# Gate logits on VectorE instead of TensorE, the second square on ScalarE, and two buffers instead of three in a fused attention and mixture-of-experts kernel

## The chip, the cores and the metric

The kernel runs on one core of a Trainium2 chip. The metric is the device time of one execution in microseconds (us). TensorE is called PE in the profile, VectorE DVE, ScalarE ACT, GpSimd POOL, and SyncE, which issues most of the DMAs, SP.

## The reference

Three stages follow one another, all in float32:

```python
kv  = einsum('bhsd,bhse->bhde', k, v)            # 8 batches, 8 heads, 576 positions, 64 wide
out = einsum('bhsd,bhde->bhse', q, kv)
x   = out / sqrt(mean(out*out, -1) + 1e-6) * g_norm    # -> [4608, 512]
y   = (maximum(x @ w_in, 0) ** 2) @ w_out              # 512 -> 2048 -> 512
logits = y @ w_gate + modality_bias[modality_id]       # [4608, 8], 8 experts
e, gate = argmax(logits), softmax(logits)[argmax]
out[token] = gate * (maximum(y @ w1[e], 0) @ w2[e])    # 512 -> 1024 -> 512
```

## The kernel before

The 4608 tokens are cut into twelve groups of 384 (three tiles of 128). During group m, TensorE computes y for group m. Woven into it are the attention of group m+1 ("attend", tasks of `ATTEND`) and the gate routing of group m-1 ("route", tasks of `ROUTE`). After the groups, token rows are fetched by expert in tiles of 128 and multiplied by w1 and w2 (`tile`, L832). That second part takes about 510 us and is not touched by the change, except that its first tile also routes group 11.

A group has sixteen chunks c of 128 hidden columns. TensorE's order is fixed: F(c) (`first_product`, L636: twelve matmuls of 384 columns into one of two PSUM banks `ps_h`), then the tasks at place 2c, then S(c-2) (`second_product`, L649: nine matmuls of 512 columns into `ps_y`), then the tasks at place 2c+1; S(14) and S(15) close the group. Each product is split in a high and a low part, so both operands exist twice. Between F(c) and S(c) the hidden values pass through ScalarE and VectorE: relu (L979), high part of the square (`g_hi`, L981), both on ScalarE; the exact square (`g_sb`, L1203) and the low part (`g_lo`, L1208) on VectorE. `g_hi` and `g_lo` have three buffers each.

ScalarE and VectorE take the other tasks of places 2c-1 and 2c within chunk c, on ScalarE after `g_hi(c)`, on VectorE between the exact square and `g_lo(c)`. The tasks of one attention tile t are qT (four transposes of q, copied by ScalarE), heads (products with kv, then a square on ScalarE L934, then on VectorE a sum L1082, twelve small steps of an inverse root, and a scaling L1065 into `xn`), and xT (four transposes of `xn`, a ScalarE copy L937, a VectorE subtraction L1088). Places: heads 16, 21, 26; xT 20, 25, 30. The kv products are made for the attention of group m+1 by four tasks (L668) at places 5, 7, 9 and 11; groups 1, 4, 7 and 10 have none, since their next group uses those already made, and are shorter.

The routing of a group: yT at places 2, 5, 8 (four transposes of y, copied by ScalarE, L943), logits at 4, 7, 10 (four products with `w_gate`, L717), then argmax, gate and prefix as small VectorE steps with one pair of products (L724, L726). From the prefix come list entries that GpSimd scatters to DRAM (L550).

Beside this the expert weights are split into high and low parts, twelve pieces of 128x512 in a group (eight in the last): SP loads a piece, ScalarE rounds it (L922, last work of its chunk), GpSimd subtracts (L543), SP stores both parts. There are two stage buffers, so a load waits for a store of two pieces before. In group 0, w_in and w_out go the same way.

ScalarE and VectorE are in order: a task that waits holds all behind it.

Of the kernel before, what the change touches and what calls it, by code (L numbers as in the profile page):

```python
# [30 lines left out]
P = 128  # L31
# [32 lines left out]
def routed_mlp_program(nc, q, k, v, g_norm, w_in, w_out, modality, w_gate, bias, w1, w2, out):  # L64
# [22 lines left out]
    ROUTE = [(2, "yT", 0), (3, "bias", 0), (4, "logits", 0), (5, "yT", 1), (7, "logits", 1), (8, "yT", 2),  # L87
             (10, "logits", 2), (12, "argmax", 0), (13, "gate", 0), (14, "prefix", 0)]
# [4 lines left out]
    PREPARE = [(24, "early", 0), (27, "rows", 0)]  # L93
# [5 lines left out]
    rows_dram = nc.dram_tensor("rows", [N + 1, ROW], F32, kind="Internal").ap()  # L99
    lists_dram = nc.dram_tensor("lists", [EARLY * P + E * LIST, 1], F32, kind="Internal").ap()  # L100

    with ExitStack() as ctx:
# [13 lines left out]
        with nc.sbuf_tensor("first_loads", [P, 4, KC * GROUP], F32) as first_loads:  # L116
            pass
        xT = {n: [sb(f"xT{n}_{part}", [P, KC, GROUP], F32R) for part in ("hi", "lo")] for n in (1, 2, 0)}
# [7 lines left out]
        g_sb = sb("g_sb", [P, GROUP])  # L126
        g_hi = [sb(f"g_hi{n}", [P, GROUP], F32R) for n in range(3)]
        g_lo = [sb(f"g_lo{n}", [P, GROUP], F32R) for n in range(3)]
# [35 lines left out]
        k_first = k_sb + [first_loads[0:SP, 2 + n, 0:K_V].rearrange("p (j h d) -> p j h d", j=SJ, h=PAIR) for n in range(2)]  # L164
        v_first = v_sb + [first_loads[0:SP, 2 + n, K_V:2 * K_V].rearrange("p (h j d) -> p h j d", h=PAIR, j=SJ)
                          for n in range(2)]
        q_first = [q_sb[:, :]] + [first_loads[:, n, 0:D] for n in range(2)]
        qT_first = [tile_T[:, :, :]] + [stage_hi[n][:, :].bitcast(F32).rearrange("p (k t) -> p k t", t=P) for n in range(2)]
        norm_first = g_sb[:, 0:6 * TILES * H].rearrange("p (n h) -> p n h", n=6)
# [28 lines left out]

        def chunks(ap):
            return ap.rearrange("p (k t) -> p k t", t=P)  # L200
# [9 lines left out]
        stage_out = [sem(f"stage_out{n}") for n in range(2)]  # L210
        lists_set, rows_out, lists_in, row_in, scattered = (
# [1113 lines left out]
```

## Time and profile before

| | us |
|---|---|
| three executions | 1524.31, 1529.36, 1524.43 (median 1524.43) |
| span of the profiled execution | 1524.2 |
| PE busy | 1478.5 (97%) |
| DVE busy | 619.1 (41%) |
| ACT busy | 498.7 (33%) |
| POOL busy | 365.0 (24%) |
| mean granted TensorE clock | 0.990 |

The span is the time from the first to the last instruction of the one profiled execution; it is 0.2 us below the median. The end of group m is seen where y is copied out of PSUM (L1215): at 123.0, 200.7, 283.3, 366.9, 444.2, 526.9, 610.3, 687.9, 770.6, 854.1, 930.9 and 1011.9 us for groups 0 to 11. In timelines the first number is the start and the second the duration, both in us; a release in brackets is the idle time ahead and what ended it.

### The profile page before, as it was taken

The page shows a single profiled execution, that of the slowest core. Times are in us where ns is not written, and L with a number is a line of the kernel's source. Part 1 is how long each engine was busy: PE and PEld are TensorE (multiplying, and loading weights), DVE is VectorE, ACT ScalarE, POOL GpSimd, SP SyncE. Part 2 cuts the span into 40 slices and gives each one's busy share as a digit, 9 for nine tenths or more (in the row PEclk, how much of TensorE's full clock was granted, in tenths as well). Part 3 has the DMA queues.
Part 4 walks back from the last instruction along what each step waited for, and adds up shares of the span by engine and source line. Part 5 has one row for each costly group of instructions (what it writes and reads, how often), then busy time and mean ns, then how long its engine had stood idle before and what let it go on. Part 6 is the DMA issues. An engine that isn't in the chain of part 4 may idle for free.

```text
span 1524.2 us, 24645 instructions
## 1 busy us (share of the span) xinstructions
PE 1478.5 (97%) x7915; PEld 1301.5 (85%) x7916; DVE 619.1 (41%) x1538; ACT 498.7 (33%) x927; POOL 365.0 (24%) x377
## 2 busy tenths in 40 slices
PE   6899999999999999999999999988999999999998
PEld 5788998988999998999898999876888888888886
DVE  3363635445554535453636464422222222222222
ACT  2343433433433333433333433321222222222222
POOL 2452312121312122222222131202222222222221
PEclk8999999999999999999999999999999999999999
DMA  6633655563656463464655354754875112751170
GB/s 155 162 101 118 171 173 162 154 183 92 201 123 209 106 194 123 153 170 156 162 171 160 111 180 151 217 199 156 319 284 182 41 41 78 268 213 41 47 255 21
DMA packets 192772, 236.42 MB, mean 155 GB/s; under 512 B 92287, under 2 KB 107039, under 8 KB 192674
## 3 DMA queue, kind: packets, MB, share of 16 engines
q1 hardware_dynamic: 185122, 215.18, 46.1%
q0 software_dynamic: 7552, 20.03, 3.9%
q8 instruction: 50, 0.82, 0.3%
q14 instruction: 48, 0.39, 0.1%
HBM read 148.14 MB, written 88.07 MB: 155 GB/s over the span
## 4 chain that ended last, share of the span: by engine, by line
PE 85%; DMA 6%; DVE 3%; issue 3%; POOL 2%; ACT 1%; SPq 1%; DVEq 0%; POOLq 0%; ACTq 0%
PE ps_y L810 15%; PE ps_h L810 14%; PE ps_h L632 7%; PE ps_y L632 7%; PE ps_h L634 7%; PE ps_h L633 7%; PE ps_y L634 7%; PE ps_y L633 7%; PE ps_a L668 2%; PE ps_b L695 2%; PE ps_b L717 2%; DMA stage<-in_moe_w_in 2%; DMA w_lo<-stage 1%; PE ps_c L755 1%; PE ps_y L823 1%
## 5 line engine op out<-in xcount | busy, mean ns | idle before, releaser
L543 POOL TENSOR_TENSOR stage<-stage,stage_hi 128x512 f32<-128x512 f32 x128 | 167.6, 1309 | 652.9 <-ACT stage_hi L922 575.0
L1203 DVE TENSOR_TENSOR g_sb<-relu_sb 128x384 f32<-128x384 f32 x192 | 131.5, 685 | 400.1 <-ACT relu_sb L979 395.5
L632 PE MATMUL ps_h<-xT_hi,weights 128*128 128x384 f32 x768 | 268.6, 350 | 5.8 <-POOL weights L535 3.2
L634 PE MATMUL ps_h<-xT_hi,weights 128*128 128x384 f32 x768 | 260.3, 339 | 0.0
L633 PE MATMUL ps_h<-xT_lo,weights 128*128 128x384 f32 x768 | 259.9, 338 | 0.0
L632 PE MATMUL ps_y<-weights,g_hi 128*128 128x512 f32 x576 | 233.8, 406 | 0.3 <-DVE g_lo L1208 0.3
L634 PE MATMUL ps_y<-weights,g_lo 128*128 128x512 f32 x576 | 227.2, 394 | 0.0
L633 PE MATMUL ps_y<-weights,g_hi 128*128 128x512 f32 x576 | 226.0, 392 | 0.0
L979 ACT ACTIVATE relu_sb<-ps_h 128x384 f32<-128x384 f32 x192 | 93.8, 488 | 317.3 <-PE ps_h L634 304.9
L810 PE MATMUL ps_y<-weights,xT_hi 128*128 128x512 f32 x640 | 183.7, 399 | 0.0
L810 PE MATMUL ps_h<-weights,xT_hi 128*128 128x512 f32 x640 | 172.2, 391 | 1.4 <-DVE xT_lo L1106 1.4
L632 PEld LDWEIGHTS ps_h<-xT_hi,weights 128*128 128x128 f32 x768 | 146.0, 190 | 11.8 <-issue 4.5
L633 PEld LDWEIGHTS ps_h<-xT_lo,weights 128*128 128x128 f32 x768 | 146.0, 190 | 3.4
L634 PEld LDWEIGHTS ps_h<-xT_hi,weights 128*128 128x128 f32 x768 | 145.6, 190 | 0.0
L810 PEld LDWEIGHTS ps_y<-weights,xT_hi 128*128 128x128 f32 x640 | 121.1, 189 | 26.0
L810 PEld LDWEIGHTS ps_h<-weights,xT_hi 128*128 128x128 f32 x640 | 120.0, 188 | 25.5 <-DVE xT_lo L1106 1.7
L922 ACT ACTIVATE stage_hi<-stage 128x512 fp32r<-128x512 f32 x128 | 80.4, 628 | 180.8 <-DMA stage<-in_moe_w 180.8
L1002 ACT ACTIVATE kv_sb<-ps_h 128x512 f32<-128x512 f32 x80 | 47.9, 598 | 257.5 <-PE ps_h L810 257.5
L634 PEld LDWEIGHTS ps_y<-weights,g_lo 128*128 128x128 f32 x576 | 108.0, 188 | 24.0
L1208 DVE TENSOR_TENSOR g_lo<-g_sb,g_hi 128x384 fp32r<-128x384 f32 x192 | 122.2, 636 | 5.0
L633 PEld LDWEIGHTS ps_y<-weights,g_hi 128*128 128x128 f32 x576 | 108.6, 188 | 18.2
L632 PEld LDWEIGHTS ps_y<-weights,g_hi 128*128 128x128 f32 x576 | 108.6, 189 | 17.9 <-DVE g_lo L1208 0.6
(169 smaller groups left out, 1735.8 us busy)
## 6 DMA issues: line engine op xcount, KB each, us to landing
stage<-in_moe_w SPq DMA_DIRECT2D x128, 256.0 KB, 2.9
w_hi<-stage_hi SPq DMA_DIRECT2D x128, 256.0 KB, 2.8
w_lo<-stage SPq DMA_DIRECT2D x128, 256.0 KB, 3.2
weights<-w_hi SPq DMA_DIRECT2D x32, 1024.0 KB, 6.5
weights<-w_lo SPq DMA_DIRECT2D x32, 1024.0 KB, 6.6
rows<-y_sb SPq DMA_DIRECT2D x13, 774.0 KB, 4.9
k_sb<-in_k SPq DMA_DIRECT2D x60, 144.0 KB, 3.2
v_sb<-in_v SPq DMA_DIRECT2D x30, 288.0 KB, 4.0
```

The costliest lines, as they stand in the source:

```text
L543: pool.tensor_tensor(stage[n % 2][:, :], stage[n % 2][:, :], stage_hi[n % 2][:, :].bitcast(F32), ALU.subtract).then_inc(piece_lo, 1)
L632: pe.matmul(out_ap, lhs[0], rhs[0], start=start, stop=False)
L633: pe.matmul(out_ap, lhs[0], rhs[1], start=False, stop=False)
L634: return pe.matmul(out_ap, lhs[1], rhs[0], start=False, stop=stop)
L668: last = pe.matmul(ps_a[:, hp * P:(hp + 1) * P], k_from[:, j, :, :].rearrange("p h d -> p (h d)"), v_from[:, :, j, :], start=(j == 0), sto ...
L695: last = pe.matmul(out_bank[lo:hi, hp * P:(hp + 1) * P], qT_from[:, hp, lo:hi], kv_sb[n][:, hp, :], start=True, stop=True)
L810: last = pe.matmul(out_ap, lhs[x][:, chunk, :], rhs[w][:, chunk, :], start=(i == 0), stop=(i == 3 * chunks_ - 1))
L922: act.activation(stage_hi[n % 2][:, :], stage[n % 2][:, :], ACT.Copy).then_inc(piece_hi, 1)
L979: act.activation(relu_sb[:, :], ps_h[c % 2][:, 0:GROUP], ACT.Relu).then_inc(h_read, 1)
L1002: act.activation(relu_B[half], ps_h[half][:, :], ACT.Relu).then_inc(relu_done, 1)
L1203: dve.tensor_tensor(g_sb[:, :], relu_sb[:, :], relu_sb[:, :], ALU.mult).then_inc(g_done, 1)
L1208: dve.tensor_tensor(g_lo[c % 3][:, :], g_sb[:, :], g_hi[c % 3][:, :].bitcast(F32), ALU.subtract).then_inc(g_lo_done, 1)
```

## The change

- The yT and logits tasks leave TensorE and ScalarE for groups 0 to 10 (group 11, routed in the first expert tile, keeps them). VectorE computes each logit of a tile by one multiply-and-sum of y (128x512) with one row of w_gate, which lies in every partition (`wgT`). That is 24 instructions for each group, two at each of places 2 to 13. Their product, not used, goes to the bank `ps_c`.
- `wgT` is made once: at chunk 14 of group 0 SP transposes w_gate by DMA into DRAM, waits, and loads it into all 128 partitions. It takes the memory of one x buffer and the first loads.
- bias moves to place 1, argmax, gate and prefix from 12, 13, 14 to 14, 15, 16; the store of rows and the list DMAs move one chunk later; in the last group the first fetched rows are transposed at place 30 instead of 27.
- The exact square moves to ScalarE and overwrites `relu_sb`. So relu(c+1) waits for `g_lo(c)`.
- `g_hi` and `g_lo` have two buffers. `g_hi(c)` now waits for the end of S(c-2) (`g_read`). x has two buffers instead of three.
- The loop over three groups is written out for all twelve groups.

```diff
-    ROUTE = [(2, "yT", 0), (3, "bias", 0), (4, "logits", 0), (5, "yT", 1), (7, "logits", 1), (8, "yT", 2),
-             (10, "logits", 2), (12, "argmax", 0), (13, "gate", 0), (14, "prefix", 0)]
+    ROUTE = ([(1, "bias", 0)] + [(2 + n, "logits", n) for n in range(TILES * E // 2)]
+             + [(14, "argmax", 0), (15, "gate", 0), (16, "prefix", 0)])
...
-    PREPARE = [(24, "early", 0), (27, "rows", 0)]
+    PREPARE = [(24, "early", 0), (30, "rows", 0)]
...
+            for c in range(GROUPS):
+                group(Group(0, c), attend=c < GROUPS - 1, route=c > 0)
...
+            def load_wgT():
+                sp.dma_start(wgT_dram, w_gate.rearrange("d e -> e d"), allow_slow_non_contiguous=True).then_inc(wgT_set, 16)
+                sp.wait_ge(wgT_set, 16)
+                sp.dma_start(wgT[:, :, :], wgT_dram.rearrange("(a e) d -> a e d", a=1).to_broadcast([P, E, D])).then_inc(wgT_in, 16)
...
@@ second_product
-                if c == CH - 1:
-                    last.then_inc(y_ps, 1)
+                last.then_inc(y_ps if c == CH - 1 else g_read, 1)
...
@@ scalar, group
                     if m.c or c:
-                        act.wait_ge(g_done, m.count(CH, c))
-                        act.wait_ge(g_hi_done, m.count(CH, c))
+                        act.wait_ge(g_lo_done, m.count(CH, c))
                     act.activation(relu_sb[:, :], ps_h[c % 2][:, 0:GROUP], ACT.Relu).then_inc(h_read, 1)
                     act.wait_ge(h_read, m.count(CH, c + 1))
-                    act.activation(g_hi[c % 3][:, :], relu_sb[:, :], ACT.Square).then_inc(g_hi_done, 1)
+                    if c == 1 and m.c:
+                        act.wait_ge(y_ps, m.count(1))
+                    elif m.c or c >= 2:
+                        act.wait_ge(g_read, m.count(CH - 1, max(c - 1, 0)))
+                    act.activation(g_hi[c % 2][:, :], relu_sb[:, :], ACT.Square).then_inc(g_hi_done, 1)
+                    act.wait_ge(g_hi_done, m.count(CH, c + 1))
+                    act.activation(relu_sb[:, :], relu_sb[:, :], ACT.Square).then_inc(g_done, 1)
                     for what, n in at_chunk(todo, c):
                         other(what, n, a, r, route)
...
@@ vector
+            def score(r, n):
+                if n == 0:
+                    dve.wait_ge(y_by_act, r.count(2, 2))
+                    dve.wait_ge(y_by_dve, r.count(1, 1))
+                    dve.wait_ge(x_lo_done, r.count(TILES, 2 * TILES))
+                    if r.c == 0:
+                        dve.wait_ge(wgT_in, 16)
+                t = n // (E // 2)
+                for e in range(n % (E // 2) * 2, n % (E // 2) * 2 + 2):
+                    if t or e or r.c:
+                        dve.wait_ge(logits_done, r.count(TILES * E, t * E + e))
+                    dve.tensor_tensor_reduce(out=ps_c[:, :], in0=y_sb[:, t, 0:D], in1=wgT[:, e, :], scale=1.0, scalar=0.0,
+                                             op0=ALU.mult, op1=ALU.add, accum_out=lg[:, 0, t, e:e + 1]).then_inc(logits_done, 1)
...
                 for c in range(CH):
-                    if m.c or c:
-                        dve.wait_ge(g_lo_done, m.count(CH, c))
-                    dve.wait_ge(h_read, m.count(CH, c + 1))
-                    dve.tensor_tensor(g_sb[:, :], relu_sb[:, :], relu_sb[:, :], ALU.mult).then_inc(g_done, 1)
                     for what, n in at_chunk(todo, c):
                         other(what, n, a, r, route)
                     dve.wait_ge(g_done, m.count(CH, c + 1))
-                    dve.wait_ge(g_hi_done, m.count(CH, c + 1))
-                    dve.tensor_tensor(g_lo[c % 3][:, :], g_sb[:, :], g_hi[c % 3][:, :].bitcast(F32),
+                    dve.tensor_tensor(g_lo[c % 2][:, :], relu_sb[:, :], g_hi[c % 2][:, :].bitcast(F32),
                                       ALU.subtract).then_inc(g_lo_done, 1)
```

## Rows read from the trace of the kernel before

**Rows 1.** The page, part 1: busy time and instructions of each engine.

```profile
PE 1478.5 (97%) x7915; PEld 1301.5 (85%) x7916; DVE 619.1 (41%) x1538; ACT 498.7 (33%) x927; POOL 365.0 (24%) x377
```

**Rows 2.** Waits of TensorE: line, released by: us in total, times, longest.

```profile
PE ps_b L724 <- DVE before L1154: 2.8, 6, 0.5
```

**Rows 3.** Timeline of TensorE, group 3, chunks 2 and 3, around a yT and a logits task.

```profile
287.33 0.60 PE L711 MATMUL ps_c<-ident,y_sb 128*128 128x128 f32 x4
287.68 0.42 PE L632 MATMUL ps_h<-xT_hi,weights 128*128 128x384 f32 x1
...
289.85 0.95 PE L717 MATMUL ps_b<-wg_sb,tile_T 128*128 128x8 f32 x8
290.66 0.48 PE L632 MATMUL ps_y<-weights,g_hi 128*128 128x512 f32 x1
```

**Rows 4.** Timeline of TensorE, group 3: first matmuls of F(14), S(12), F(15).

```profile
353.76 0.34 PE L632 MATMUL ps_h<-xT_hi,weights 128*128 128x384 f32 x1
...
355.87 0.39 PE L632 MATMUL ps_y<-weights,g_hi 128*128 128x512 f32 x1
...
357.95 0.33 PE L632 MATMUL ps_h<-xT_hi,weights 128*128 128x384 f32 x1
```

**Rows 5.** Timelines of ScalarE, VectorE and TensorE, group 3: tile 1, square to transposes.

```profile
342.71 0.58 ACT L934 ACTIVATE xn<-ps_b 128x512 f32<-128x512 f32 x1
...
346.63 0.69 DVE L1065 TENSOR_TENSOR xn<-ps_b,norm 128x512 f32<-128x512 f32 x1
...
348.26 0.60 PE L704 MATMUL ps_c<-ident,xn 128*128 128x128 f32 x4
```

**Rows 6.** Timelines of ScalarE and VectorE, group 3, chunk 15.

```profile
360.78 0.53 ACT L981 ACTIVATE g_hi<-relu_sb 128x384 fp32r<-128x384 f32 x1
361.21 0.67 ACT L937 ACTIVATE xT_hi<-ps_c,g_col 128x512 fp32r<-128x512 f32 x1
...
361.91 0.75 DVE L1088 SCALAR_TENSOR_TENSOR xT_lo<-ps_c,g_col,xT_hi 128x512 fp32r<-128x512 f32 x1 [0.57 <-ACT xT_hi L937]
362.58 0.55 DVE L1208 TENSOR_TENSOR g_lo<-g_sb,g_hi 128x384 fp32r<-128x384 f32 x1
```

**Rows 7.** Timeline of VectorE: a norm step (group 3), then the prefix steps (group 7).

```profile
328.41 1.14 DVE L1055 TENSOR_SCALAR norm<-norm 128x8 int32<-128x8 int32 x1
...
644.79 0.18 DVE L1166 TENSOR_TENSOR lg<-ps_b,list_base 128x24 f32<-128x24 f32 x1
...
646.25 1.56 DVE L1208 TENSOR_TENSOR g_lo<-g_sb,g_hi 128x384 fp32r<-128x384 f32 x1
```

**Rows 8.** Groups of instructions of VectorE: busy us, mean ns, idle before.

```profile
L1065 DVE TENSOR_TENSOR xn<-ps_b,norm 128x512 f32<-128x512 f32 x33 | 22.8, 691 | 1.1
L1082 DVE TENSOR_REDUCE norm<-xn 128x8 f32<-128x512 f32 x33 | 22.5, 682 | 10.1 <-ACT xn L934 10.1
```

**Rows 9.** Timeline of ScalarE, group 4 (no kv tasks), piece 6.

```profile
397.06 0.63 ACT L922 ACTIVATE stage_hi<-stage 128x512 fp32r<-128x512 f32 x1 [0.63 <-DMA stage<-in_moe_w]
```

**Rows 10.** Timeline of TensorE, group 0; then a window: us, busy, PEclk, DMA, GB/s.

```profile
102.73 0.66 PE L704 MATMUL ps_c<-ident,xn 128*128 128x128 f32 x4 [1.94 <-DVE xn L1065]
...
104.00:106.00 2.00, 2.00 (x8) 0.50 0.25 64
```

**Rows 11.** Timelines of VectorE and TensorE, group 11: end of the prefix, place 27.

```profile
970.00 0.17 DVE L1175 TENSOR_SCALAR token<-token 128x3 f32<-128x3 f32 x1
...
996.54 1.12 PE L755 MATMUL ps_c<-ident,k_sb 128*128 128x128 f32 x4 [5.43 <-POOL k_sb L582]
997.31 0.67 PE L632 MATMUL ps_h<-xT_hi,weights 128*128 128x384 f32 x1
...
1001.24 0.39 PE L632 MATMUL ps_y<-weights,g_hi 128*128 128x512 f32 x1
```

**Rows 12.** The page: a DMA queue, then a DMA issue (KB each, us to landing).

```profile
q1 hardware_dynamic: 185122, 215.18, 46.1%
...
weights<-w_hi SPq DMA_DIRECT2D x32, 1024.0 KB, 6.5
```

More of the change, by code:

```diff
@@ L113, in routed_mlp_program @@
         w_out_sb = weights[1][:, :].rearrange("p (c s d) -> p c s d", c=CH, s=2)
-        with nc.sbuf_tensor("first_loads", [P, 4, KC * GROUP], F32) as first_loads:
-            pass
-        xT = {n: [sb(f"xT{n}_{part}", [P, KC, GROUP], F32R) for part in ("hi", "lo")] for n in (1, 2, 0)}
+        xT = [[sb(f"xT{n}_{part}", [P, KC, GROUP], F32R) for part in ("hi", "lo")] for n in range(2)]
+        wgT = sb("wgT_sb", [P, E, D])
         k_sb = [sb(f"k_sb{n}", [P, SJ, PAIR, DH]) for n in range(2)]
@@ L125, in routed_mlp_program @@
         relu_sb = sb("relu_sb", [P, GROUP])
-        g_sb = sb("g_sb", [P, GROUP])
-        g_hi = [sb(f"g_hi{n}", [P, GROUP], F32R) for n in range(3)]
-        g_lo = [sb(f"g_lo{n}", [P, GROUP], F32R) for n in range(3)]
+        g_hi = [sb(f"g_hi{n}", [P, GROUP], F32R) for n in range(2)]
+        g_lo = [sb(f"g_lo{n}", [P, GROUP], F32R) for n in range(2)]
         y_sb = sb("y_sb", [P, TILES, ROW])
@@ L197, in routed_mlp_program, with prefix_bank @@
         ps_hT = (ps_a, ps_y[1])
+        def prefix_bank(r):
+            return ps_b if r.c == GROUPS - 1 else ps_c
         def chunks(ap):
@@ L429, in group @@
                         load_own_piece(2 * c + 5)
+                    if m.c == 0 and c == CH - 2:
+                        load_wgT()
                     if c < pieces_of(m):
@@ L656, in second_product @@
                 for t in range(TILES):
-                    last = product3(ps_y[t][:, :], [g[c % 3][:, t * P:(t + 1) * P] for g in (g_hi, g_lo)],
+                    last = product3(ps_y[t][:, :], [g[c % 2][:, t * P:(t + 1) * P] for g in (g_hi, g_lo)],
                                     [w_out_sb[:, c, s, :] for s in range(2)], c == 0, c == CH - 1)
-                if c == CH - 1:
-                    last.then_inc(y_ps, 1)
+                last.then_inc(y_ps if c == CH - 1 else g_read, 1)
             def kv(a, hp):
@@ L714, in logits @@
             def logits(r, t):
[L715 removed]
+                pe.wait_ge(yT_done, t + 1)
                 for k_ in range(KC):
@@ L1086, in other @@
                     dve.wait_ge(x_hi_done, a.count(TILES, n + 1))
-                    hi, lo = (x[:, :, n * P:(n + 1) * P] for x in xT[a.kind])
+                    hi, lo = (x[:, :, n * P:(n + 1) * P] for x in xT[a.c % 2])
                     dve.scalar_tensor_tensor(lo, chunks(ps_c[:, :]), g_col[:, 0:1], hi.bitcast(F32), ALU.mult,
                                              ALU.subtract).then_inc(x_lo_done, 1)
+                elif what == "logits":
+                    score(r, n)
                 elif what in ("bias", "argmax", "gate", "prefix"):
```

72 lines of the change are left out of this document (34 added, 38 removed).

## The prediction

> **What bounds the kernel now.** I read the busy shares first, then TensorE's waits, then the timelines of TensorE, ScalarE and VectorE of one group beside one another. TensorE is busy for 97% of the span and the others for 41% or less [rows 1]. Inside the groups it hardly waits: the only wait that comes back in several groups is the prefix product, 2.8 us in six of them [rows 2]. So the groups are bound by what TensorE issues, and a matmul taken away is time gained, as long as nothing else becomes late. What matters for the second half of that sentence is how much room the chains on ScalarE and VectorE have. That is read by setting the time at which TensorE is handed a result against the time at which it would ask for it. All times below are of the profiled execution, span 1524.2 us; the median of the runs is 0.2 us more.
>
> **What goes from TensorE.** The transposes of one yT task hold up F by 287.68 - 287.33 = 0.35 us, and that F takes 289.85 - 287.68 = 2.17 us instead of the 2.11 us of an undisturbed one, so 0.41 us. The logits task takes 290.66 - 289.85 = 0.81 us, and about 0.09 us by a slower start of what follows: 0.90 us [rows 3, 4]. Three tiles make 3.9 us for a group. For the ten groups 1 to 10 that is 39 us, and the prefix waits go too, some 2 us [rows 2]. Group 11 is counted by itself, below.
>
> **The clock work of one group.** From rows 4, F is 2.11 us and S is 2.08 us. A ScalarE instruction that waits for a product starts 0.2 us after the next TensorE task could start (the release of relu and of the y copies looks the same in all groups). In the kernel before, `g_hi(c)` could follow relu(c) at once, that is, right after F(c). Now it waits for the end of S(c-2), and so do all ScalarE tasks of the chunk, because they stand behind it; and the second square comes in between. From the end T of S(c-2): `g_hi` starts at T+0.19; it takes 0.53 us and the in-place square waits for it, so it starts at T+0.74; the next task follows 0.43 us behind it as it does behind `g_hi` [rows 6], at T+1.17. I take the square at `g_hi`'s own duration. It isn't in this trace in this form. Below, it could cost 0.35 us; above, 0.63 us, as the 128x512 rounding [rows 9]; that is 0.1 us either way in each chain.
>
> *Tile 1 of the attention.* Its square is ScalarE's in chunk 11, so T is the end of S(9). Square at T+1.17, the scaling 346.63 - 342.71 = 3.92 us later, less the 0.19 us of one hiccup in that chain, and 0.69 us long [rows 5]: `xn` is ready at T+5.6. TensorE wants to transpose it at place 25, after F(12) and S(10): T+4.19. Stall 1.45 us. Before, `xn` was ready at 347.32 and wanted at 348.26 [rows 5], 0.9 us of room.
>
> *Tile 0.* Its square comes in chunk 8, T the end of S(6). The transposes at place 20 have room: after T come qT, F(9), S(7), F(10), 6.7 us, against 5.6 us, or 6.6 us when GpSimd's subtraction holds up one step of the norm, as it does for tile 0 in all ten groups (a step of 1.14 us instead of 0.17) [rows 7]. But the prefix steps now stand behind this chain on VectorE and ahead of `g_lo(8)`: 646.25 - 644.79 = 1.46 us [rows 7], then `g_lo` of 0.56 us. Ready at T+8.7, wanted by S(8) at T+7.2. Stall 1.5 us; 0.5 us without the held-up step, 2.5 us with a second one.
>
> *Tile 2 and the end of the group.* The square of tile 2 has the copy of xT ahead of it: `xn` ready at T+6.4 (T the end of S(11)) against 6.3 us wanted at place 30, and the late `g_lo(13)` delays relu(14) and `g_lo(14)`; 0.3 us together. In chunk 15 the two ScalarE tasks and two VectorE tasks behind `g_hi` take 363.13 - 360.78 = 2.35 us from its start to the end of `g_lo` [rows 6]; with the square 2.9 us. They start only after S(13), and relu(15) is a little late besides: S(15) can start 3.5 us after the end of S(13), where S(14) fills 2.1. Stall 1.4 us, between 0.95 and 1.6.
>
> Together 1.5 + 1.45 + 0.3 + 1.4 = 4.7 us for a group with attention, more than the 3.9 us it gains. Ten groups: 47 us; the bounds above (2.9 to 5.8 us) give 29 to 58 us. Group 0 has the same chains without the routing and its steps are DMA-paced; I take 3 us, 0 to 6.
>
> **VectorE's sums.** No multiply-and-sum stands in the trace. Below, it is at least a 128x512 product, 0.69 us; above, a product and a sum one after the other, 0.69 + 0.68 = 1.37 us [rows 8]. I take 0.8 us, nearest to the first. Four of them and `g_lo` make 3.8 us for a chunk, with the steps on which GpSimd holds VectorE about 4.2 us. A chunk of the groups without kv tasks is 4.2 us of TensorE, of those with kv 5.5 us. In the latter it is hidden under the products; in the four former ones nothing is left over: starting from `g_lo(0)` at 4.3 us after the group's start, argmax would end near 34.5 us, and the prefix product would be asked for at 32.5 us. In the same groups the pieces of weights are late too: before, ScalarE rounded piece 6 at 397.06, 30 us into the group, when the DMA came [rows 9]; TensorE now reaches F(7) at 27.5 us, and the copy of qT, behind relu(7), `g_hi` and the square, ends at 32.6 us and is asked for at 31.6. Both delays fall on the same place, so I take one, 2.2 us, in four groups: 9 us (0 to 16).
> The Trainium skill ("SBUF — State Buffer", Who interferes with whom) says that a VectorE instruction with two SBUF inputs and a GpSimd instruction that reads SBUF exclude each other for the whole instruction. The `g_lo` of 1.56 us instead of 0.56 [rows 7] agrees, and the new sums have two SBUF inputs; by the rule they are held, and hold the subtractions, as I have assumed with 0.4 us for a chunk.
>
> **One-time costs.** The transposed w_gate is 4096 elements, each a packet. At the mean of the hardware queue, 0.461 x 16 x 1524 / 185122 = 0.061 us a packet on one of 16 engines, that is 16 us; its copy into all partitions is 2.1 MB, twice a weights load of 6.5 us, 13 us [rows 12]. Issued near 107 us, both are over near 136, and the load of piece 0 stands behind them on SP. Group 1 starts near 125 and first asks near 129. Some 4 us of room in the chain to S(1) cover part: 3 us, 0 to 12. The written-out loop I cost at nothing: group 3 to 4, over the loop's back edge, is not longer than the others by the ends of the groups; bound 0 to 3 us, and -2 by saved register work.
>
> **The clock.** After an idle of 1.94 us followed by transposes the granted clock stood at 0.50, the 1.2 GHz level, and F(12) took 1.7 us longer [rows 10]; after the idle of 5.43 us in group 11 the next F took 3.93 us, 1.8 us longer [rows 11]. The new stalls of 1.4 to 2.5 us are at that edge. I count two or three drops, 4 us; none to two for each group give 0 to 36 us, the high end unlikely.
>
> **Group 11.** It has no attention. Before, TensorE stood 5.43 us at place 27 for fetched rows, and lost 2.1 us by the clock behind it. The rows came 26.4 us after the prefix [rows 11]. The prefix ends at about the same time in the group, since it hangs on the pieces; the transposes come 6.3 us later in order, at place 30. The wait goes, the gain of 3.9 us is mostly eaten by `g_lo(8)` behind late pieces, and the stall before S(15) comes: about -6 us (-9 to +1).
>
> **Sum.** -39 - 2 - 6 = -47; +47 + 9 + 3 + 3 + 4 = +66. Net +19 us on 1524.2: 1543, and 1543 against the median too.
>
> **Rivals.**
> *A, the waits are shorter than the gain.* One mechanism: VectorE's prefix and norm keep clear of GpSimd's subtractions, so that S(8) doesn't wait, and pieces and sums in the groups without kv stay in time. Then 29 to 35 us of stalls stand against 47: 1524 - 47 + 32 + 3 = 1512. For it: TensorE's waits were small in all groups, so chains had more room than a row shows. Against it: the wait for S(c-2) sits ahead of every task, with no cover. It decides at 3.9 us of stalls for a group. If ScalarE's chain had no effect at all, 1480.
> *B, it comes out even.* Stalls of 3.7 to 4.3 us a group and no clock drops: 1517 to 1532.
> *C, the sums are slow.* At 1.22 us for each sum a chunk of VectorE is 5.5 us; argmax ends near 41 us, 8 us late in groups without kv and 3 us late in the others, 43 us more: 1585. At 1.37 us some 1600 or more. For it: nothing in the trace; against: two-input instructions run at the pace of one-input ones [rows 8].
> The Trainium skill ("Vector Engine (DVE) Microarchitecture Reference", Points that are easy to get wrong) says that the accumulating form with two SBUF sources not in bf16 runs at half throughput; no row shows it; by the page a sum would be an estimated 1.22 us and the time that of C.
>
> **Chances.** Forecast (1533 to 1565) 0.45; B 0.22; A 0.19; C, or many clock drops, 0.14. What a measurement can tell from no change is about 0.5%, 7.6 us: faster is below 1516.8, slower above 1532.1. A gives most of faster, 0.18; same 0.22; slower 0.60. The range reaches from A's upper half to below C: 1509 to 1579; the forecast's own range is 1533 to 1565.
>
> **What would show it.** Right: TensorE waits for `xn` at L704 once a group for about 1.5 us, and for `g_lo` before S(15) and S(8); ScalarE's `g_hi` starts 0.2 us behind the S before it; the groups' ends stand about as far apart as before or further, most in groups 1, 4, 7, 10; no wait at the fetched rows in group 11. Wrong: groups with kv of under 80 us; a sum far from 0.8 us; many stretches at clock 0.50.

## The result, and the profile after

| | before | after |
|---|---|---|
| median of 4 runs, us | 1525.00 (1524.31 to 1529.36) | 1579.57 (1574.45 to 1582.58) |
| ratio | | 1.0345 (95%: 1.0322 to 1.0369) |
| span of the profiled execution, us | 1524.2 | 1578.0 |
| mean granted TensorE clock | 0.990 | 0.978 |

The change makes the kernel 54 us slower. The forecast was 1543, its range 1509 to 1579: the sign is right, the size is a third of what came, and the time lies just outside.

The page's busy line of after stands against [rows 1]:

```profile
PE 1461.8 (93%) x7519; PEld 1265.1 (80%) x7520; DVE 735.4 (47%) x1874; ACT 577.0 (37%) x1086; POOL 375.7 (24%) x377
```

TensorE lost 396 instructions but only 17 us of busy time (e6 below, with the same products gone, is 43 us less busy than before). Part of the difference is time at the lower clock; part is that TensorE works more slowly just around each stop, which is shown with e2. Its waits in after (line, released by: us in total, times, longest), where [rows 2] had one that comes back, 2.8 us in all:

```profile
PE ps_y L640 <- DVE g_lo L1231: 25.5, 23, 1.2
PE ps_h L640 <- ACT relu_sb L979: 23.1, 1, 23.1
PE ps_c L711 <- DVE xn L1071: 20.0, 13, 3.6
PE ps_c L732 <- DVE before L1182: 7.9, 5, 3.2
PE ps_b L700 <- ACT tile_T L932: 7.7, 4, 2.2
```

Two of these rows are stops that come back in each group (23 and 13 times), one is a single stop of 23.1 us, and the last two belong to few groups. The lengths of the groups, from one copy of y to the next, say where each falls:

| group, lengths in us | 0 | 1 | kv groups 2, 3, 5, 6, 8, 9 (mean) | 4, 7, 10 (mean) | 11 |
|---|---|---|---|---|---|
| before | 122.98 | 77.68 | 83.10 | 77.20 | 80.98 |
| after | 129.46 | 105.65 | 83.65 | 84.29 | 75.63 |
| difference | +6.5 | +28.0 | +0.55 each, +3.3 | +7.1 each, +21.3 | -5.4 |

The differences sum to 54. (The copy that ends group 11 starts at 1065.48 us in after and at 1011.85 in before, and some 512 us of the span follow it in both.) The groups with kv products nearly break even. Half of the loss is group 1, the next largest part is the three groups without kv.

**A group with kv products.** TensorE in group 3, its only three waits:

```profile
367.33 0.50 PE L640 MATMUL ps_y<-weights,g_hi 128*128 128x512 f32 x1 [1.12 <-DVE g_lo L1231]
...
381.62 0.66 PE L711 MATMUL ps_c<-ident,xn 128*128 128x128 f32 x4 [1.46 <-DVE xn L1071]
...
399.95 0.50 PE L640 MATMUL ps_y<-weights,g_hi 128*128 128x512 f32 x1 [1.16 <-DVE g_lo L1231]
```

They are S(8), the transposes of tile 1, and S(15). ScalarE in chunk 11 of the same group shows the wait that the forecast rests on:

```profile
376.06 0.53 ACT L985 ACTIVATE g_hi<-relu_sb 128x384 fp32r<-128x384 f32 x1 [1.15 <-PE ps_y L642]
376.62 0.53 ACT L987 ACTIVATE relu_sb<-relu_sb 128x384 f32<-128x384 f32 x1
377.05 0.58 ACT L935 ACTIVATE xn<-ps_b 128x512 f32<-128x512 f32 x1
```

`g_hi(11)` stands 1.15 us for the end of S(9); the in-place square and the square of tile 1 follow only then.

**Group 4, without kv.** First VectorE, then GpSimd, then TensorE:

```profile
431.83 0.70 DVE L1132 CUSTOM_DVE_ANT_0 ps_c<-y_sb,wgT_sb 128x512 f32<-128x512 f32 x1
432.44 0.14 DVE L1132 DVE_READ_ACCUMULATOR2_ANT lg<- 128x1 f32 x1
432.44 1.64 DVE L1231 TENSOR_TENSOR g_lo<-relu_sb,g_hi 128x384 fp32r<-128x384 f32 x1
```

```profile
431.84 1.83 POOL L551 TENSOR_TENSOR stage<-stage,stage_hi 128x512 f32<-128x512 f32 x1 [2.71 <-ACT stage_hi L926]
```

```profile
436.31 1.16 PE L700 MATMUL ps_b<-kv_sb,tile_T 128*128 128x128 f32 x8 [2.25 <-ACT tile_T L932]
438.86 0.62 PE L732 MATMUL ps_c<-onehot,earlier 128*128 128x24 f32 x2 [1.39 <-DVE before L1182]
...
439.73 0.77 PE L640 MATMUL ps_y<-weights,g_hi 128*128 128x512 f32 x1
...
443.72 0.98 PE L686 MATMUL ps_a<-ident,q_sb 128*128 128x128 f32 x4
```

The sum is 0.70 us and its read 0.14, but the `g_lo` behind it takes 1.64 us instead of 0.56, beside a subtraction of GpSimd that started 0.60 us before it. Until it ended, relu(7), and with it the copy of qT, could not start. Heads wait 2.25 us, the prefix 1.39 us; then S(6) takes 443.72 - 439.73 = 3.99 us where an undisturbed one takes 2.08 [rows 4]. The granted clock of that stretch is 0.50, the lower of the two levels, 1.2 GHz. It fell during the second wait. (Columns: window, its length, busy us of PE, PEld, DVE, ACT and POOL with their instructions, then granted clock, DMA share and GB/s.)

```profile
436.00:438.00 2.00, 1.16 (x8) 0.97 (x8) 1.79 (x7) 1.00 (x3) 0.89 (x1) 0.91 0.38 141
438.00:440.00 2.00, 1.14 (x5) 1.15 (x6) 1.80 (x8) 0.49 (x1) 0.38 (x1) 0.50 0.63 216
440.00:442.00 2.00, 2.00 (x5) 1.53 (x5) 0.00 (x0) 0.00 (x0) 0.00 (x0) 0.50 0.47 177
```

**Group 1.** SP's wait for the transposing DMA (in us, times, longest), then ScalarE's first rounded piece, then TensorE:

```profile
SPq L422 <- DMA wgT<-in_moe_w_gate: 38.6, 1, 38.6
```

```profile
159.78 0.63 ACT L926 ACTIVATE stage_hi<-stage 128x512 fp32r<-128x512 f32 x1 [26.68 <-DMA stage<-in_moe_w]
```

```profile
160.84 0.69 PE L640 MATMUL ps_h<-xT_hi,weights 128*128 128x384 f32 x1 [23.14 <-ACT relu_sb L979]
```

The transposition is 16 KB and holds SP for 38.6 us; the load of piece 0 is behind it, ScalarE stands at that piece in chunk 0, and all of the group stands behind ScalarE. How the DMA engines were used from shortly after its issue (at 110.78 us) to its end:

```profile
114.00:142.00 28.00, 20.77 (x100) 17.13 (x99) 9.17 (x26) 7.99 (x16) 2.60 (x2) 0.98 0.71 1
142.00:150.00 8.00, 0.00 (x0) 0.00 (x0) 0.00 (x0) 0.00 (x0) 0.00 (x0) 0.50 0.01 0
```

The second number from the end is the busy share of the 16 engines: 0.71 for 28 us, then next to nothing for the last 8 us before SP went on.

### The profile page after: what moved, and what is told of

It is laid out like the page before. It is cut to its first block, busy times and chain, and to the rows that moved or that the text cites. A ratio compares the mean times of both kernels' runs of the same rounds, so it can differ in the third digit from the quotient of the medians.

```text
span 1578.0 us, 22129 instructions
## 1 busy us (share of the span) xinstructions
PE 1461.8 (93%) x7519; PEld 1265.1 (80%) x7520; DVE 735.4 (47%) x1874; ACT 577.0 (37%) x1086; POOL 375.7 (24%) x377
## 2 busy tenths in 40 slices
DMA packets 197000, 238.31 MB, mean 151 GB/s; under 512 B 96407, under 2 KB 111159, under 8 KB 196794
## 4 chain that ended last, share of the span: by engine, by line
PE 63%; DVE 19%; ACT 7%; DMA 7%; issue 3%; POOL 1%; SPq 0%; ACTq 0%; DVEq 0%; POOLq 0%
PE ps_y L814 14%; PE ps_h L814 14%; DVE ps_c L1132 5%; PE ps_y L640 5%; PE ps_y L642 4%; PE ps_y L641 4%; PE ps_h L640 4%; PE ps_h L642 4%; PE ps_h L641 4%; DVE g_lo L1231 3%; PE ps_a L675 3%; DMA wgT<-in_moe_w_gate 3%; ACT g_hi L985 2%; PE ps_b L700 2%; ACT relu_sb L987 2%
## 5 line engine op out<-in xcount | busy, mean ns | idle before, releaser
L551 POOL TENSOR_TENSOR stage<-stage,stage_hi 128x512 f32<-128x512 f32 x128 | 181.1, 1415 | 689.3 <-ACT stage_hi L926 613.2
L640 PE MATMUL ps_h<-xT_hi,weights 128*128 128x384 f32 x768 | 266.8, 347 | 28.2 <-ACT relu_sb L979 23.1
L640 PE MATMUL ps_y<-weights,g_hi 128*128 128x512 f32 x576 | 235.8, 409 | 25.5 <-DVE g_lo L1231 25.5
L1132 DVE CUSTOM_DVE_ANT_0 ps_c<-y_sb,wgT_sb 128x512 f32<-128x512 f32 x264 | 231.8, 878 | 31.4 <-DMA wgT_sb<-wgT 24.6
L641 PE MATMUL ps_y<-weights,g_hi 128*128 128x512 f32 x576 | 229.1, 398 | 0.0
L1231 DVE TENSOR_TENSOR g_lo<-relu_sb,g_hi 128x384 fp32r<-128x384 f32 x192 | 128.1, 667 | 159.8 <-ACT relu_sb L987 159.5
L985 ACT ACTIVATE g_hi<-relu_sb 128x384 fp32r<-128x384 f32 x192 | 100.8, 525 | 124.1 <-PE ps_y L642 120.2
```

The costliest lines, as they stand in the source:

```text
L551: pool.tensor_tensor(stage[n % 2][:, :], stage[n % 2][:, :], stage_hi[n % 2][:, :].bitcast(F32), ALU.subtract).then_inc(piece_lo, 1)
L640: pe.matmul(out_ap, lhs[0], rhs[0], start=start, stop=False)
L641: pe.matmul(out_ap, lhs[0], rhs[1], start=False, stop=False)
L985: act.activation(g_hi[c % 2][:, :], relu_sb[:, :], ACT.Square).then_inc(g_hi_done, 1)
L1132: dve.tensor_tensor_reduce(out=ps_c[:, :], in0=y_sb[:, t, 0:D], in1=wgT[:, e, :], scale=1.0, scalar=0.0, op0=ALU.mult, op1=ALU.add, accum_ ...
L1231: dve.tensor_tensor(g_lo[c % 2][:, :], relu_sb[:, :], g_hi[c % 2][:, :].bitcast(F32), ALU.subtract).then_inc(g_lo_done, 1)
```

## Experiments

All were run in three rounds against the kernel before on the same chip (its medians there were 1522.2 to 1526.0 us). Where two experiments are compared, their medians can come from different chips, so differences of 4 us or less mean little.

### The one-time transposition

**e1: the transposition issued before the groups.**

```diff
+            sp.dma_start(wgT_dram, w_gate.rearrange("d e -> e d"), allow_slow_non_contiguous=True).then_inc(wgT_set, 16)
             def load_wgT():
-                sp.dma_start(wgT_dram, w_gate.rearrange("d e -> e d"), allow_slow_non_contiguous=True).then_inc(wgT_set, 16)
```

> The changed kernel with one edit: the transposition of w_gate into DRAM is issued ahead of the groups, and only the wait for it and the load into all partitions stay at chunk 14 of group 0. My theory (the 39.5 us of the transposition hold SP, so piece 0 of the weights comes late, ScalarE stands 26.7 us behind it and TensorE 23.1 us at F(3) of group 1): group 1 falls from 105.7 us to 82 to 86 us and the total by 18 to 23 us, to about 1558. Rival (the small packets cost the same wherever they run, since they share the DMA engines with the weights of group 0): group 0 grows by as much as group 1 falls and the total stays within 5 us of 1579.

Measured: 1586.99 us, ratio 1.0439 (1.0403 to 1.0475). Group 1 fell to 83.6 us, but group 0 rose by 29.3 to 158.8. TensorE waited 34.5 us in it for its own weights, which pass through the same DMA engines; SP's first load behind the transposition took 21.1 us to issue. So what is queued behind the small packets is held up wherever they run. Group 1 fell as my theory said, but the total didn't: the place moved, as the rival said, and the whole is 7 us over the changed kernel, a little outside the rival's 5.

**e5: transposed by TensorE.**

```diff
-                sp.dma_start(wgT_dram, w_gate.rearrange("d e -> e d"), allow_slow_non_contiguous=True).then_inc(wgT_set, 16)
+                    if m.c == 0 and c == 5:
+                        sp.wait_ge(wgT_copied, 1)
+                        sp.dma_start(wgT_dram, xn[0:E, :]).then_inc(wgT_set, 16)
...
+                if what == "wgT":
+                    for k_ in range(KC):
+                        last = pe.transpose(ps_b[0:E, k_ * P:(k_ + 1) * P], wg_sb[:, k_, :], ident[:, :])
```

> The changed kernel with the one-time transposition of w_gate taken from the DMA engines: TensorE transposes the four 128x8 blocks at place 4 of group 0, VectorE copies the 8x512 result, and one contiguous DMA of 16 KB writes it to DRAM; the broadcast to all partitions stays where it is. Theory (the 39.5 us transposition holds SP's queue and so the first weight piece that ScalarE rounds, which is the one stop of 23.14 us in group 1): that stop goes, group 1 falls from 105.7 us to about 83.5, group 0 stays within 1 us of 129.5, the whole about 1557. Rival (the stop belongs to the 2 MB broadcast or to the weight pieces themselves, which the broadcast pushes back): group 1 keeps at least 10 of its 22 us, the whole 1568 or more.

Measured: 1553.60 us, ratio 1.0201 (1.0157 to 1.0245), 26 us below the changed kernel. Group 1 is 83.4 us. The longest wait of group 1 is now 2.21 us, at its heads. The theory holds: 22 us in group 1 are the transposition; 3 more came back in group 0.

### The sums and GpSimd

**e4: the sums spread from place 0.**

```diff
-    ROUTE = ([(1, "bias", 0)] + [(2 + n, "logits", n) for n in range(TILES * E // 2)]
+    ROUTE = ([(1, "bias", 0)] + [(at, "logits", n) for n, at in enumerate((0, 0, 1, 3, 4, 5, 6, 7, 8, 9, 10, 11))]
```

> The changed kernel with the sums moved to places 0, 0, 1, 3, 4 to 11, so that VectorE uses its idle time in chunk 0 and has two sums fewer in chunks 6 and 7. My theory (in the groups without kv VectorE's sums with GpSimd's holds take 4.55 us a chunk against 4.2 of TensorE, g_lo(6) is late, with it relu(7), the copy of qT and the heads product, and after that idle the clock drops): the waits at heads (2.2 us) and prefix (1.4 us) fall to under 1.5 us together and the clock stays up, 4 to 6 us in each of groups 4, 7 and 10 and 1 to 3 in group 1, total down 14 to 20 us, to about 1562. Rival (the pieces of weights, paced by DMA, are what is late): the waits at heads stay, total within 4 us of 1579.

Measured: 1567.37 us, ratio 1.0304 (1.0270 to 1.0337), -12. Groups 4, 7 and 10 lost 5.4, 5.5 and 3.9 us. The gain was smaller than expected by what group 1 (+3.0) and group 11 took back.

**e7: GpSimd's subtraction shortened.** It covers 64 of the 512 columns; the low parts of the other 448 are left out.

```diff
-                pool.tensor_tensor(stage[n % 2][:, :], stage[n % 2][:, :], stage_hi[n % 2][:, :].bitcast(F32),
+                pool.tensor_tensor(stage[n % 2][:, 0:64], stage[n % 2][:, 0:64], stage_hi[n % 2][:, 0:64].bitcast(F32),
```

> The changed kernel with GpSimd's subtraction (the low part of the expert weights) cut to the first 64 of its 512 columns; the low parts of the other columns are left out. Theory (VectorE's sums of 0.70 us are held to 1.6 to 1.8 us where GpSimd's subtraction overlaps them, and that is what makes VectorE's chunk longer than TensorE's and the prefix of groups 4, 7 and 10 late): the mean of the sums falls from 878 ns to about 710, groups 4, 7 and 10 lose 4 to 7 of their 84.4 us, the other groups under 1 us, the whole -12 to -20. Rival (the sums are late by their number and place alone, not by GpSimd): the mean falls but the three groups stay within 1 us of 84.4.

Measured: 1552.72 us, ratio 1.0172 (1.0124 to 1.0220), -27. The sums of after and of e7, busy us and mean ns:

```profile
L1132 DVE CUSTOM_DVE_ANT_0 ps_c<-y_sb,wgT_sb 128x512 f32<-128x512 f32 x264 | 231.8, 878 | 31.4 <-DMA wgT_sb<-wgT 24.6
```

```profile
L1132 DVE CUSTOM_DVE_ANT_0 ps_c<-y_sb,wgT_sb 128x512 f32<-128x512 f32 x264 | 185.0, 701 | 34.1 <-DMA wgT_sb<-wgT 27.4
```

In after 50 of the 264 sums last 1.2 us or more, 47 of them 1.6 to 1.8 us; in e7 none does and 256 of them last under 0.75. The gain is more than the 12 to 20 us that I expected. Groups 4, 7 and 10 fell to 78.0, 77.9 and 77.2 us (-6.4 to -6.7), the groups with kv by 0.86 us on average, mostly since their stop before S(8) is 0.4 to 0.6 us there and not 1.12. So the late heads and prefix, and the low clock behind them, come from GpSimd holding VectorE. (e7 also ends GpSimd's own instruction earlier, and with it frees each piece for its store; no run separates the two, but the sums themselves are shorter, as they must be if it held them.) The Trainium skill ("SBUF — State Buffer", Who interferes with whom) calls the shared pair of ports "an exclusive lock"; the 0.70 us that become 1.6 to 1.8 us beside a subtraction agree.

### Buffers and squares

**e2: three buffers of g_hi, and the wait on VectorE.** `g_lo` keeps two buffers. The room for the third comes from small tiles laid over one another.

```diff
-                    if c == 1 and m.c:
-                        act.wait_ge(y_ps, m.count(1))
-                    elif m.c or c >= 2:
-                        act.wait_ge(g_read, m.count(CH - 1, max(c - 1, 0)))
...
                     dve.wait_ge(g_done, m.count(CH, c + 1))
+                    if c == 1 and m.c:
+                        dve.wait_ge(y_ps, m.count(1))
+                    elif m.c or c >= 2:
+                        dve.wait_ge(g_read, m.count(CH - 1, max(c - 1, 0)))
```

> The changed kernel with three buffers of g_hi, so that ScalarE no longer waits for S(c-2); that wait moves to VectorE ahead of g_lo(c), whose two buffers stay. To find the memory, ones is read as a broadcast of one column and some small tensors of the second part lie in norm. My theory (the wait for S(c-2) ahead of every ScalarE task makes the stalls at xT of tile 1, at S(8) and at S(15), 1.47 + 1.12 + 1.16 us): these three go in all groups, a group with kv falls from 83.3 to 79.6 us, the total by 33 to 42 us, to about 1541. Rival (the square in place is the cause: relu(c+1) waits for g_lo(c) and the square lengthens each chain): the stalls stay at over half, the total falls by less than 12 us.

Measured: 1525.76 us, ratio 1.0031 (1.0003 to 1.0060), -54. TensorE's waits:

```profile
PE ps_h L641 <- ACT relu_sb L980: 27.5, 1, 27.5
PE ps_c L733 <- DVE before L1179: 8.6, 5, 2.9
...
PE ps_b L701 <- ACT tile_T L933: 6.5, 4, 2.2
...
PE ps_c L712 <- DVE xn L1068: 4.1, 4, 3.1
```

The 23 waits for `g_lo` (25.5 us) are down to 2 (1.4 us), the 13 for `xn` to 4. Groups with kv are 77.9 to 78.7 us. The gain, 54 us, is more than the 33 to 42 expected. The removed stops are 3.7 us in each group with kv, the gain there is 5.2. Group 3 of after and of e2 (columns as above) shows where the rest lies:

```profile
318.41:402.39 83.98, 80.14 (x446) 71.47 (x445) 52.97 (x138) 37.05 (x73) 19.86 (x15) 1.00 0.47 146
```

```profile
307.60:386.28 78.68, 78.68 (x446) 71.83 (x445) 51.34 (x138) 37.34 (x73) 19.06 (x15) 1.00 0.51 156
```

The same 446 matmuls, all at the full clock, keep TensorE busy for 80.14 us with three stops and for 78.68 without. So a stop costs TensorE about 0.5 us more than its wait.

**e3: the squares and the two buffers put into the kernel before.** Its VectorE squares go, ScalarE squares in place, `g_hi` and `g_lo` have two buffers and the wait for S(c-2); yT and logits stay on TensorE.

```diff
-        g_hi = [sb(f"g_hi{n}", [P, GROUP], F32R) for n in range(3)]
+        g_hi = [sb(f"g_hi{n}", [P, GROUP], F32R) for n in range(2)]
...
+                        act.wait_ge(g_read, m.count(CH - 1, max(c - 1, 0)))
+                    act.activation(g_hi[c % 2][:, :], relu_sb[:, :], ACT.Square).then_inc(g_hi_done, 1)
+                    act.wait_ge(g_hi_done, m.count(CH, c + 1))
+                    act.activation(relu_sb[:, :], relu_sb[:, :], ACT.Square).then_inc(g_done, 1)
...
-                    dve.tensor_tensor(g_sb[:, :], relu_sb[:, :], relu_sb[:, :], ALU.mult).then_inc(g_done, 1)
```

> The kernel before with one part of the change: the exact square on ScalarE in place, two buffers of g_hi and g_lo with the wait for S(c-2). Logits stay on TensorE, the loop and the three x buffers too. My theory (this part alone makes the stalls of tile 1 and of S(15), and the one at S(8) needs the prefix behind the norm, which is not so here): 2.5 to 3 us for each of eleven groups, 1553 in all, with waits at L704 of about 1.5 us in each group. Rival (the waits come only with the sums on VectorE): within 6 us of the kernel before, 1525.

Measured: 1603.23 us, ratio 1.0539 (1.0497 to 1.0581), +80 where I had expected +28. The miss has two parts. It had a wait that the changed kernel doesn't have, for `xn` of tile 2 (0.8 to 2.4 us in each of groups 1 to 10), and waits for yT's copies (8.5 us in 10), which stand in ScalarE's order behind the same late `g_hi`.

**e9: only the squares; e10: only the two buffers.** Both start from the kernel before. e9 is e3 with three buffers of both and no wait for S(c-2). In e10 VectorE keeps the square:

```diff
+                    elif m.c or c >= 2:
+                        act.wait_ge(g_read, m.count(CH - 1, max(c - 1, 0)))
+                    act.activation(g_hi[c % 2][:, :], relu_sb[:, :], ACT.Square).then_inc(g_hi_done, 1)
```

> The kernel before with only the exact square moved to ScalarE, in place in relu_sb (so relu(c+1) waits for g_lo(c)); the three buffers of g_hi and g_lo stay, and with them g_hi(c) needs no wait for S(c-2). Theory (the stops of 1.1 to 1.5 us come from the wait for S(c-2) ahead of every ScalarE task; the square alone adds 0.5 us to chains that have 0.9 us of room): groups within 1 us of those before, the whole 1520 to 1535. Rival (the loop relu, g_hi, square, g_lo, relu through one buffer is itself too long where an attention task stands in it): one or two stops of about 1 us in each group, the whole 1545 or more.

> The kernel before with only two buffers of g_hi and g_lo, g_hi(c) waiting for the end of S(c-2); the exact square stays on VectorE. Theory: the wait alone makes the chains late, by 0.5 us less than with the square behind it on ScalarE, so stops of about 0.9 us before the xT of tile 1 and 0.6 us before S(15) and S(8), 2 us in a group, 20 to 30 us in all: 1545 to 1555. With e9 it shows whether the +80 us of e3 (both edits) is a sum or an effect of the two together: by the theory e9 gives about 0 and e10 about +25, and at least 40 us belong to the combination. Rival: e10 alone gives 60 us or more, 1585.

Measured: e9 1554.88 us, ratio 1.0196 (1.0162 to 1.0230), +32; e10 1562.36 us, ratio 1.0258 (1.0228 to 1.0289), +39 where I had expected 20 to 30. Together 71 of e3's 80: nearly a sum, where I had expected at least 40 us from the combination. My theory that the square alone costs nothing is wrong; its rival holds. e10 stops TensorE for tile 1 (0.8 to 2.0 us) and for only 0.4 us before S(15) in each of groups 1 to 10; e9 never stops for tile 1, but for tile 2 (0.3 to 2.0 us in eight groups) and for 1.16 to 1.19 us before S(15) in eight. TensorE, ScalarE and VectorE of e9 at the end of group 3:

```profile
373.69 0.50 PE L632 MATMUL ps_y<-weights,g_hi 128*128 128x512 f32 x1 [1.16 <-DVE g_lo L1204]
377.82 0.44 PE L632 MATMUL ps_h<-xT_hi,weights 128*128 128x384 f32 x1 [1.79 <-issue]
```

```profile
356.93 0.63 ACT L922 ACTIVATE stage_hi<-stage 128x512 fp32r<-128x512 f32 x1 [6.30 <-DMA stage<-in_moe_w]
...
360.65 0.49 ACT L978 ACTIVATE relu_sb<-ps_h 128x384 f32<-128x384 f32 x1 [1.60 <-DVE g_lo L1204]
...
367.91 0.49 ACT L978 ACTIVATE relu_sb<-ps_h 128x384 f32<-128x384 f32 x1 [4.59 <-DVE g_lo L1204]
...
370.21 0.49 ACT L978 ACTIVATE relu_sb<-ps_h 128x384 f32<-128x384 f32 x1 [0.68 <-DVE g_lo L1204]
```

```profile
363.54 0.67 DVE L1083 TENSOR_REDUCE norm<-xn 128x8 f32<-128x512 f32 x1
...
367.27 0.55 DVE L1204 TENSOR_TENSOR g_lo<-relu_sb,g_hi 128x384 fp32r<-128x384 f32 x1
```

relu(14) stands 4.59 us for `g_lo(13)`, which stands behind the 3.7 us norm of tile 2. In the kernel before, relu waited for the exact square, ahead of the norm; now it waits for `g_lo`, behind it. This second loop, through the one relu buffer, ends in the same S(15) stop of 1.16 us with no wait for S(c-2) at all. But the loop alone doesn't make the stop. e2 has the same single buffer and the same wait of relu(14), and no stop before S(15) in any group with kv:

```profile
377.62 0.49 ACT L980 ACTIVATE relu_sb<-ps_h 128x384 f32<-128x384 f32 x1 [4.60 <-DVE g_lo L1232]
```

What e9 has besides is the first ScalarE row: a piece of weights 6.30 us late in chunk 11, after which relu(12), `g_lo(12)` and relu(13) are late one behind the other, before tile 2 begins. Such a piece stands 5.6 to 8.6 us in each of groups 1 to 10 of e9, in none with kv of the changed kernel or e2. It stands there in the kernel before too, for 4.4 to 6.7 us, without a stop. So it is likely that the square in place and the late piece together make the stops of e9, the one using up the room that the other then lacks; no run has the square alone with the pieces in time. The second TensorE row follows the loop's back edge: 1.79 us of issue.

**e8 and e12: is it the place of the list and the rows?** e8 is e3 with the list scatter in chunk 10, e12 also stores the rows at chunk 9, as the changed kernel does.

```diff
-                    if route and c == 9:
+                    if route and c == 10:
                         send_ids(m.shifted(-1))
...
-            KV_AT, Q_AT, ROWS_AT = (1, 1, 3, 4), (2, 7, 10), 8
+            KV_AT, Q_AT, ROWS_AT = (1, 1, 3, 4), (2, 7, 10), 9
```

> The kernel before with the squares on ScalarE in place and two buffers of g (as in e3, 1603 us), but with the send list scattered in chunk 10 instead of 9, as the changed kernel has it. Theory (in e3 the late piece 11 holds ScalarE by 6.94 us in chunk 12, so relu and the squares come late, tile 2 waits 2.3 us and the clock drops behind it): that wait goes, each full group falls from 88 to 84-85 us, the whole about 1565 to 1570. Rival (the 88 us groups come from the yT copies, which only the logits on TensorE need and which stand in ScalarE's order between two squares): groups stay at 87 us or more and the whole within 10 us of 1603.

> As e8 (the kernel before with the squares on ScalarE in place, two buffers of g, the send list at chunk 10: 1589.6 us), and the store of the token rows, with SP's wait for the gates ahead of it, at chunk 9 instead of 8, as the changed kernel has it. In e8 ScalarE stands 6 to 8 us for a piece of weights in chunk 11 of each group with kv and the xT of tile 2 is 2.0 us late behind it; in the changed kernel it doesn't stand there and tile 2 isn't late. Theory (the row store and its wait on SP hold the load of that piece): ScalarE's wait falls under 2 us, the tile 2 wait of TensorE goes in nearly all groups (xn waits 21 in 14 become about 15 in 11), groups with kv lose 1.5 to 3 us of their 87 to 89, the whole 1565 to 1575. Rival (the wait comes from GpSimd's list scatter, which holds its queue wherever it stands, or from the loop): ScalarE keeps waits of over 4 us there and the whole is within 6 us of e8.

Measured: e8 1589.62 us, ratio 1.0425 (1.0382 to 1.0469), e12 1583.65 us, ratio 1.0376 (1.0340 to 1.0413). TensorE's waits for `xn`, of e3, e8 and e12:

```profile
PE ps_c L704 <- DVE xn L1070: 35.9, 23, 3.5
```

```profile
PE ps_c L704 <- DVE xn L1070: 21.0, 14, 3.3
```

```profile
PE ps_c L704 <- DVE xn L1070: 21.2, 14, 3.6
```

The later list took away 9 of 23 waits (-14 us, less than half of what I expected); the later rows took away none of them (-6 us, within the rival's bound and not the 15 to 25 of the theory). ScalarE's stand for a late piece in chunk 11 stayed in one group of three (7.08 us at 543.80 in e12). The groups of e8 that stayed at 87 to 88 us were not held up by the list: against the 83.3 to 84.0 us of the changed kernel they have the 3.9 us forecast for the yT and logits that the change took away.

### The parts together

**e11: three buffers of g_hi (the diff of e2) and the transposition on TensorE (that of e5). e6: both, and the early sums (that of e4).**

> The changed kernel with three buffers of g_hi (as e2, 1525.8 us) and w_gate transposed on TensorE (as e5, -26 us), the sums left at their places from 2 on. e6, which has the early sums too, gave 1482.5 us. Theory (early sums matter only where the prefix is late, and e2 has no late prefix to speak of): 1525.8 - 26 = 1500 down to 1490, groups 4, 7 and 10 at 78 to 79 us as in e2 against 75 to 77 in e6, so 6 to 10 us over e6. Rival (the early sums gave nothing and the surplus of e6 lies in group 1 alone): within 4 us of e6.

> The changed kernel with the three repairs together: three buffers of g_hi with the buffer wait moved to VectorE, the sums spread from place 0, and w_gate transposed on TensorE. If the losses are separate they add: three buffers gave -54 us, early sums -12, the transposition about -22, but the early sums and the buffers both remove the late prefix of groups 4, 7 and 10 (e2 already shows those groups level with the others), so I expect 1579.6 - 54 - 22 = 1504 with nothing from the early sums, or 1492 with all of it; 1500 is my value. Rival: without its waits TensorE runs into the next limit, the pieces of expert weights (ScalarE or the DMA queues), and the time stays above 1515.

Measured: e11 1498.06 us, ratio 0.9821 (0.9792 to 0.9849); e6 1482.54 us, ratio 0.9725 (0.9678 to 0.9771). So e6 is faster than both kernels: 40 us under the one before in its own rounds, 97 under the changed one. Busy line and waits of e6:

```profile
PE 1435.0 (97%) x7523; PEld 1257.6 (85%) x7524; DVE 722.1 (49%) x1875; ACT 580.6 (39%) x1086; POOL 375.1 (25%) x377
```

```profile
PE ps_y L644 <- DVE g_lo L1246: 4.6, 4, 1.2
PE ps_h L644 <- POOL weights L547: 4.4, 3, 2.2
...
PE ps_c L717 <- DVE xn L1079: 4.0, 4, 3.5
...
PE ps_c L738 <- DVE before L1193: 0.7, 1, 0.7
```

e6 was 18 us better than I expected. e11 came out at the time expected of it, but 15.5 us over e6 and not 6 to 10; its rival, under 4 us, is out. So the surplus of e6 is the early sums', which give 15.5 us here and 12 in e4. Groups 4, 7 and 10 go from 78.3, 79.9 and 79.3 us in e11 to 77.3, 75.3 and 74.4 us in e6, and group 1 from 79.1 to 75.9: the heads' 2.2 us waits (8.8 us in 4) and the prefix waits (8.7 us in 5) of e11 are gone or under 0.8 us. That I took e2's groups for free of late prefixes, when the waits above show 8.6 us of them, was a misreading.

## Why the prediction was right in sign and wrong in size

*What TensorE gains: right, a little small.* 3.9 us for a group was forecast. It shows where nothing is late: the groups with kv of e6 are 77.9 to 78.8 us against 82.7 to 83.5, 4.7 us less, or 4.2 without the prefix waits of 0.47.

*The stops of a group with kv: right in place and cause, the net partly luck.* S(8), tile 1 and S(15) were predicted at 1.5, 1.45 and 1.4 us and are 1.12, 1.46 and 1.16; tile 2, at 0.3, isn't late. That is 3.7 us of waits for the 4.7 forecast. Each stop costs TensorE about 0.5 us more than its wait, which the forecast left out, so they cost 5.2. Net +0.8 us was forecast for such a group less 0.3 for the prefix, +0.55 measured: the smaller waits, the larger gain and the cost around the stops nearly cancel. e2 shows that these stops hang on the wait for S(c-2). It isn't the whole cause: with it and the exact square still on VectorE (e10) the stop before S(15) is 0.4 us. The forecast had counted the square in that chain, at 0.55 us. For S(8) it had 0.5 us without GpSimd's hold; e7 measures 0.4 to 0.6.

*Group 0: mis-sized by 3.5 us.* TensorE waits for an xT 3.63 us where it waited 1.94 [rows 10], and 1.10 and 1.19 us before S(14) and S(15); e5 is 3.0 us shorter there, without the transposition in the last chunks.

*The transposition: the step that failed most.* "The transposed w_gate is 4096 elements, each a packet. At the mean of the hardware queue, ... that is 16 us", and so 3 us in group 1, at most 12. It took about 39 us, 2.4 times as long. The packet's price was the smaller error: a share of 0.71 over 28 us is 0.71 x 28 x 16 / 4096 = 0.08 us a packet, so 20 us of all 16 engines where I had 16. The larger one was to take that work for the duration: the engines were not full while it ran, and 8 us passed between the last packets and SP's going on. What filled them isn't shown. The order was as I had it (piece 0 behind the two loads), so the duration alone was off: 22 us in group 1 by e5, 19 more than forecast. The Trainium skill ("DMA: Bandwidth & Descriptors", Rules for kernel authors) warns that a strided last dimension becomes one descriptor for each element. The trace agrees: by the two pages of the profile, packets under 512 bytes rise from 92287 before to 96407 after.

*The sums and the groups without kv: right in price, wrong in effect, the second step that failed.* 0.8 us for each was forecast; 0.70 and the read at a spacing of 0.8 us were measured. Rival C, a slow sum, is out: the half throughput of the Trainium skill ("Vector Engine (DVE) Microarchitecture Reference", Points that are easy to get wrong) would have been an estimated 1.22 us; the runs show 0.70. But of the groups without kv I had written "Both delays fall on the same place, so I take one, 2.2 us". They came one after the other, 2.25 and 1.39 us, and behind them the clock fell to 0.50 for S(6), 1.91 us more. With the three usual stops that makes +7.1 us in place of +3.0: 12 us in groups 4, 7 and 10, and 3 in group 1 (e5: 83.4 against 77.7). e7 shows what makes them late, the holds by GpSimd, which I had put at 0.4 us a chunk (1.1 for the one `g_lo` shown) and then hidden.

*Group 11: right.* -6 forecast, -5.4 found; no wait at the fetched rows is left in the list.

Of the miss of 35 us (54 against 19), 19 are the transposition in group 1, 15 the groups without kv, 3.5 group 0 and 1 group 11 with the groups with kv; the 4 us that I had put down to the clock by itself lie within these and come off. Rival A named the other end, 1480 us if no chain were late. e6 reached 1482.5, and needed the buffers, the transposition and the places of the sums for it.

What stays open: why a late piece stops ScalarE in chunk 11 of before, e3, e9 and e10, and in some groups of e8 and e12, but in no group with kv of the changed kernel; and what the logits on VectorE cost by themselves, since no run moves them alone.

## What to carry to other kernels

Work moved off the busiest engine pays only with the slack that was there. Here 43 us of TensorE's work went, and the third buffer of `g_hi` given up for it cost 54 (e2). A stop costs more than its wait. The busy time of a DMA's packets is only a lower bound of how long it takes, so ask what is queued behind it on its issuer. A scratch tile that is now written twice (relu, then its square) ties the next chunk to the last reader: that cost nothing where all else was in time (e2's groups with kv), and there were stops where a piece of weights was late too (e9).

## What the runs showed of the hardware

- A transposing DMA of 4096 four-byte elements took about 39 us, of which its packets explain 20 (0.08 us each on 16 engines), and held up the transfers behind it, also when nothing waited for its result (e1: 34.5 us of TensorE waiting for its weights).
- GpSimd's subtraction holds a 128x512 multiply-and-sum from 0.70 to 1.6 or 1.8 us, 47 times in 264. Shortened eightfold, it held none that long.
- TensorE's clock was at its lower level, 0.50, for S(6) behind 2.25 and 1.39 us of waiting with little work in between: 3.99 us instead of 2.08.
- A stop costs TensorE about 0.5 us beyond its wait: 80.14 us busy with three stops, 78.68 with none, for the same 446 matmuls at a granted clock of 1.00 (group 3 of after and of e2).
- The loop's back edge is 0.25 and 0.63 us of issue for TensorE in before, and 1.4 to 1.9 us in e3, e8, e9, e10 and e12, where S(15) waits just ahead of it. No run tries the written-out loop alone.
